# Hidden layers copied ahead of the exponential, a convolution cut in two, and finer waits, in an attention, gate and mixer kernel on one core

## The reference

```python
scores = q @ k.T / 8;  mask = scores >= the 32nd largest of its row
x = softmax(scores where mask) @ v                  # heads side by side: (4, 576, 512)

gate = sigmoid(sum over k of 5: conv_w[k] * x shifted by 4-k tokens)
x = (gate * (x @ w_val)) @ w_out

mixed = real(fft(fft(x, tokens), features));  u = x + mixed
un = (u - mean) / sqrt(var + 1e-6)
out = u + relu(un @ w_ch1) @ w_ch2                  # hidden width 2048
```

## Time and profile before

| | |
|---|---|
| median of 3 runs | 1065.74 us (1063.03 to 1066.76) |
| profiled execution, time | 1062.11 us |
| profiled execution, span | 1060.3 us |
| mean granted TensorE clock | 0.965 |
| busy TensorE matmul / weight load | 972.6 us (92%) / 830.5 us (78%) |
| busy VectorE | 832.9 us (79%) |
| busy ScalarE | 644.6 us (61%) |
| busy GpSimd | 408.1 us (38%) |

### The profile page before, as it was taken

How to read it: one execution, slowest core, us unless ns; L and a number is a source line. 1 busy time by engine, 2 the same in 40 slices (tenths; PEclk the granted TensorE clock), 3 DMA queues, 4 the chain that set the end, 5 groups by cost and what they waited for, 6 DMA issues and landing times.

```text
span 1060.3 us, 20106 instructions
## 1 busy us (share of the span) xinstructions
PE 972.6 (92%) x6784; PEld 830.5 (78%) x6784; DVE 832.9 (79%) x1809; ACT 644.6 (61%) x1421; POOL 408.1 (38%) x544
## 2 busy tenths in 40 slices
PE   4887767899999999999999999899899999999997
PEld 3565656678788898788888898688788887788896
DVE  7999999998999999989998886998998963120000
ACT  5887787766677767566677565576586761122121
POOL 2675554445433233245342323254342223443221
PEclk9987887899999999999999999999999999999999
DMA  8564656550267778401878565300677766059873
GB/s 243 176 203 158 207 170 213 191 204 23 86 244 270 279 264 284 156 4 63 289 250 264 189 221 188 128 28 23 212 260 256 255 254 213 1 187 370 282 253 128
DMA packets 84549, 203.80 MB, mean 192 GB/s; under 512 B 9056, under 2 KB 30304, under 8 KB 84448
## 3 DMA queue, kind: packets, MB, share of 16 engines
q1 hardware_dynamic: 84288, 202.22, 56.3%
q10 hardware_dynamic: 160, 0.30, 0.1%
HBM read 178.89 MB, written 23.59 MB: 191 GB/s over the span
## 4 chain that ended last, share of the span: by engine, by line
PE 71%; DVE 10%; issue 8%; ACT 7%; POOL 3%; DMA 1%; SPq 0%; ACTq 0%; DVEq 0%; POOLq 0%
PE p_m L759 18%; PE p_m L744 17%; PE p_t L597 8%; PE p_s L567 6%; PE p_t L581 5%; PE p_m L608 5%; PE p_m L638 3%; PE p_m L712 3%; DVE top L973 3%; DVE rest L984 3%; PE p_m L628 2%; ACT pT L851 2%; ACT prob L837 2%; PE p_t L601 1%; ACT s_sb L825 1%
## 5 line engine op out<-in xcount | busy, mean ns | idle before, releaser
L973 DVE MAX8 top<-rest 128x8 f32<-128x576 f32 x432 | 309.9, 745 | 0.1
L1245 POOL TENSOR_TENSOR hid_lo<-hid,hid_hi 128x256 fp32r<-128x256 f32 (+1 forms) x128 | 105.2, 822 | 307.6 <-ACT hid_hi L919 307.6
L984 DVE MATCH_REPLACE8 rest<-top,rest 128x576 f32<-128x576 f32 x288 | 213.8, 742 | 0.0
L759 PE MATMUL p_m<-w_st,hid_hi 128*128 128x512 f32 x576 | 182.4, 398 | 5.7 <-POOL hid_lo L1245 5.5
L744 PE MATMUL p_m<-un_hi,w_st 128*128 128x256 f32 (+1 forms) x1024 | 164.5, 303 | 4.7 <-ACT hid_hi L919 4.6
L825 ACT ACTIVATE s_sb<-p_s 128x576 f32<-128x576 f32 x144 | 93.1, 647 | 100.3 <-PE p_s L567 100.2
L744 PEld LDWEIGHTS p_m<-un_hi,w_st 128*128 128x128 f32 x1024 | 143.0, 188 | 12.2 <-issue 8.6
L581 PE MATMUL p_t<-id_sb,prob 128*128 128x128 f32 x720 | 108.8, 283 | 26.9 <-ACT prob L843 26.8
L597 PE MATMUL p_t<-pT,v_sb 128*64 128x128 f32 (+1 forms) x1600 | 108.6, 288 | 23.7 <-ACT pT L851 23.7
L918 ACT ACTIVATE hid<-p_m 128x256 f32<-128x256 f32 (+1 forms) x128 | 51.3, 401 | 127.0 <-PE p_m L744 124.0
L597 PEld LDWEIGHTS p_t<-pT,v_sb 128*64 128x64 f32 x1600 | 89.2, 149 | 49.3 <-ACT pT L851 29.6
(11 more groups left out here) (117 smaller groups left out, 1642.1 us busy)
## 6 DMA issues: line engine op xcount, KB each, us to landing
w_st<-w_split SPq DMA_DIRECT2D x256, 512.0 KB, 4.8
w_split<-w_st SPq DMA_DIRECT2D x32, 512.0 KB, 3.1
k_raw<-kT SPq DMA_DIRECT2D x62, 144.0 KB, 3.0
q_raw<-qT SPq DMA_DIRECT2D x60, 144.0 KB, 2.9
u<-w_ch SPq DMA_DIRECT2D x32, 256.0 KB, 3.8
v_sb<-v SPq DMA_DIRECT2D x16, 256.0 KB, 3.0
w_st<-wout_split SPq DMA_DIRECT2D x16, 256.0 KB, 4.1
out<-u SPq DMA_DIRECT2D x16, 256.0 KB, 2.4
```

Of the source, the lines that this page charges most:

```text
L759: mm = pe.matmul(mbank(j), h[i % 2][:, P * j:P * j + P], w2_st[i % NB2][:, w, :], start=f == 0 and part == 0, stop=f == FC - 1 and part == 2)
L973: found = dve.max(top[t % NK][:, 8 * n:8 * n + 8], (rest[t % 2] if n else s_sb[t % NS])[:, :])
L984: chained(dve.match_replace(rest[t % 2][:, :], top[t % NK][:, 8 * n:8 * n + 8], (rest[t % 2] if n else s_sb[t % NS])[:, :], LOWEST), t)
L1245: pool.tensor_tensor(hid_lo[i % 2][:, 0:width(b, g)], hid[:, 0:width(b, g)], hid_hi[i % 2][:, 0:width(b, g)].bitcast(F32), ALU.subtract).t ...
```

## The change

It has seven parts. (1) In slots whose first step is `ch0` n with n < 12, ScalarE does that step (the two Relu copies) ahead of `exponent`. (2) GpSimd's `deviation` of r=4 moves from step `proj` 4 to behind `hid_lo` of layer 1. (3) The convolution of c = 3 is cut into columns 0 to 383 (`FRONT`, slots 39 to 41, as soon as three fifths of `x_new` are there) and 384 to 575 (`BACK`, all five taps in slot 42). (4) `zed` 2 goes to bank 3 and waits for `gv` chunk by chunk; `sequence` g=0 takes its three operands in the order in which ScalarE copies them, each with a wait of its own. (5) `values` waits for `x_new` pair by pair. (6) Layer 1 of `ch1` goes to bank 2 in odd batches too, and `sums` of layer 0 then waits for that layer's copy before it uses bank 2. (7) `w_val` is loaded 15 slots earlier.

```diff
     if g == 0:
         return 3 if f == 1 or f >= 12 and f % 2 == 0 else 2
-    return 2 if b % 2 == 0 and f % 2 else 3
+    return 2 if (b % 2 == 0 or f == 1) and f % 2 else 3
...
+ZED_BANK = [0, 1, 3]
...
-           35: [(2, (0, 1))], 36: [(2, (2, 3))], 37: [(2, (4,))], 42: [(3, (0, 1))], 43: [(3, (2, 3, 4))]}
+WHOLE, FRONT, BACK = (0, S), (0, 3 * P), (3 * P, S)
+           39: [(3, FRONT, (0, 1))], 40: [(3, FRONT, (2, 3))], 41: [(3, FRONT, (4,))], 42: [(3, BACK, range(TAPS))]}
...
-                    if i == 2 * FC - 1:
+                    if i == FC:
                         sp.dma_start(wslot[:, :, :], w_val.rearrange("(c q) n -> q c n", q=P)).then_inc(m_wval, 16)
...
                     for k in pairs:
+                        if j == 0:
+                            pe.wait_ge(s_x, 5 * (PAIRS * b + k + 1))
...
-                        pe.wait_ge(s_x, 5 * PAIRS * (b + 1))
...
                     if m == 2:
-                        pe.wait_ge(m_gv, upto_gv(b + 1, 0))
                         for k in range(KC):
+                            pe.wait_ge(m_gv, upto_gv(b, max(2 * (k + 1), 5)))
...
-                        pe.wait_ge(m_zev, 3 * b + 3)
...
+                    for n, k in enumerate((2, 0, 1)):
+                        if g == 0:
+                            pe.wait_ge(m_zev, 3 * b + n + 1)
...
                     for j in range(len(GROUPS[b % 2][g])):
+                        if f == 0 and j == 2:
+                            pe.wait_ge(m_hev, i + 2)
...
+                    first = any(what == "ch0" and n < 12 for what, b, n in plan[s][0:1])
+                    if first:
+                        step(*plan[s][0])
                     if due(s, EXPONENT):
                         exponent(s - EXPONENT)
...
-                    for x in plan[s][0:1]:
-                        step(*x)
+                    if not first:
+                        for x in plan[s][0:1]:
+                            step(*x)
...
-                    dve.wait_ge(s_x, 5 * (p + 1))
+                    n0, n1 = part
+                    dve.wait_ge(s_x, 5 * p + (3 if part == FRONT else 5))
...
-                    elif what == "proj":
+                    elif what == "proj" and n < NR - 1:
                         deviation(b, n)
...
+                        if g == 0 and n == 1:
+                            deviation(b, NR - 1)
```

More of the change, by code:

```diff
@@ L359, in conv_due @@
         def conv_due(s):
-            return [(b, c, taps) for b in range(1, B) for c, taps in CONV_AT.get(s - NT * b, [])]
+            return [(b, *x) for b in range(1, B) for x in CONV_AT.get(s - NT * b, [])]
         def tanh_due(s):
@@ L669, in zed @@
                     if m == 2:
[L670 removed]
                         for k in range(KC):
+                            pe.wait_ge(m_gv, upto_gv(b, max(2 * (k + 1), 5)))
                             for half, c0 in enumerate((0, DM - NCOS)):
[L674 removed]
+                                mm = pe.matmul(mbank(ZED_BANK[m])[LEFT * half:LEFT * half + LEFT, 0:NCOS], gv_rows(k, 4),
                                                wfeat[:, k, c0:c0 + NCOS], start=k == 0, stop=k == KC - 1,
@@ L680, in zed @@
                         for o, (c0, c1) in enumerate(((0, NCOS), (NCOS, DM))):
-                            mm = chain(mbank(m), slice(0, P), c0, c1, [folded(k, o, m) for k in range(KC)],
+                            mm = chain(mbank(ZED_BANK[m]), slice(0, P), c0, c1, [folded(k, o, m) for k in range(KC)],
                                        [wfeat[:, k, c0:c1] for k in range(KC)])
@@ L691, in sequence @@
                     cols = slice(P * g, P * g + TCH[g])
-                    for tab, c0, c1 in ((cos_sb, 0, NCOS), (sin_sb, NCOS, DM)):
-                        mm = chain(mbank(SEQ_BANK[g]), seq_rows(b, g), c0, c1, [tab[:, k, cols] for k in range(3)],
-                                   [z[:, 0, c0:c1], z[:, 1, c0:c1], z_last[:, NCOS - (c1 - c0):NCOS]])
+                    bank = mbank(SEQ_BANK[g])[seq_rows(b, g), :]
+                    for n, k in enumerate((2, 0, 1)):
+                        if g == 0:
+                            pe.wait_ge(m_zev, 3 * b + n + 1)
+                        for tab, c0, c1 in ((cos_sb, 0, NCOS), (sin_sb, NCOS, DM)):
+                            part = z_last[:, NCOS - (c1 - c0):NCOS] if k == 2 else z[:, k, c0:c1]
+                            mm = pe.matmul(bank[:, c0:c1], tab[:, k, cols], part, start=n + c0 == 0, stop=n == 2,
+                                           skip_group_check=True)
                     mm.then_inc(m_ab, 1)
@@ L1033, in reciprocal, with conv @@
                     dve.reciprocal(rinv[:, c], rinv[:, c]).then_inc(s_rinv, 1)
-                def conv(b, c, taps):
+                def conv(b, c, part, taps):
                     p = PAIRS * b + c
-                    dve.wait_ge(s_x, 5 * (p + 1))
+                    n0, n1 = part
+                    dve.wait_ge(s_x, 5 * p + (3 if part == FRONT else 5))
                     if c == 0:
@@ L1040, in conv @@
                     for k in taps:
-                        src = x_new[p % NX][:, k:k + S]
+                        to, src = gate[:, c, n0:n1], x_new[p % NX][:, k + n0:k + n1]
                         if k == 0:
-                            dve.tensor_scalar(gate[:, c, :], src, cw_sb[:, c, 0:1], None, ALU.mult).then_inc(m_conv, 1)
+                            dve.tensor_scalar(to, src, cw_sb[:, c, 0:1], None, ALU.mult).then_inc(m_conv, 1)
                         else:
                             dve.wait_ge(m_conv, tapped[0])
-                            dve.scalar_tensor_tensor(gate[:, c, :], src, cw_sb[:, c, k:k + 1], gate[:, c, :],
-                                                     ALU.mult, ALU.add).then_inc(m_conv, 1)
+                            dve.scalar_tensor_tensor(to, src, cw_sb[:, c, k:k + 1], to, ALU.mult,
+                                                     ALU.add).then_inc(m_conv, 1)
                         tapped[0] += 1
@@ L1129, in _ @@
                         low_keys(p)
-                    for b, c, taps in conv_due(s):
-                        conv(b, c, taps)
+                    for b, c, part, taps in conv_due(s):
+                        conv(b, c, part, taps)
                     for x in plan[s][1:]:
```

12 lines of the change are left out of this document (7 added, 5 removed).

## The result

| | before | changed |
|---|---|---|
| median | 1065.19 us (1063.03 to 1066.76, 4 runs) | 1049.03 us (1045.98 to 1052.33, 4 runs) |
| ratio, 95% interval | | 0.985 (0.981 to 0.989) |
| profiled execution: time, span | 1062.11, 1060.3 us | 1052.33, 1050.6 us |
| VectorE busy | 832.9 us | 839.0 us |

The changed kernel is faster by 1.5%. Repeated with the kernel before on the same chip it gave 1048.75 us (1046.24 to 1051.45, 6 runs) against 1063.36, ratio 0.987 (0.984 to 0.989), so 14.6 to 16.2 us. The two profiled executions differ by only 9.8: the changed kernel's was the slowest of its four runs, and that of the kernel before was shorter than all four of its timed runs.

A forecast was written before the change was run, and what follows sets the result against it. VectorE and TensorE were taken to bound the kernel in turn. Terms 5.0 + 2.5 + 1.0 + 5.1 + 1.9 + 0.8 + 1.1 = 17.4, taken as 17 us, gave about 1049 us; forecast between 1045 and 1053, range 1044 to 1059.

The forecast's parts named there:

- What bounds the kernel: VectorE sets 60 to 208 us, both engines are full 268 to 422, TensorE alone counts after 886.
- Deviation, 5.0, and 1.5 of clock: TensorE's waits behind GpSimd in slots 54, 126, 89 and last batch go, 5.0 us; half clock behind slot 126, 1.5.
- Order on ScalarE, net 1.0: Hidden copies ahead of the exponential: 3.5 us gained in two-layer slots, 2.5 lost to stalls in short slots.
- Convolution, 5.1, and its 1.0 of clock: Gates of batches 1 and 2: earlier taps end ScalarE's tanh wait, saving TensorE 5.1 us, plus 1.0 of half clock.
- No stretch at half clock after 680 us: Sign expected in the changed profile: TensorE's half-clock spell behind slots 115 and 116 is gone.
- VectorE's idle time as cover: Cut's extra 0.6 us per batch is covered by VectorE's 2.5 us idle from 422 us, more in slots 111 to 113.
- Finer waits: `zed` and `sequence` start by chunk or operand: 1.9 us (bounds 0 and 3.2), about 1.3 of wait remaining in batch 1.
- The sum of the parts, given as 4.7: At 454 us, batch 1: 2.0 + 0.6 - 1.2 + 1.5 + 1.9, against 3.3 us with the last chunk still waiting.
- The rest: `values` of the last batch 0.8 us, bank 2 for `ch1` layer 1 in the last batch 1.1, earlier `w_val` nothing.
- VectorE is the bound: Rival, chance 0.13: TensorE's gains in its full stretches become waits for the top-32 search; gain about 7.6, so 1058 us.
- ScalarE did not stay blocked: Rival, chance 0.12, said ScalarE stays blocked: BACK's taps and searches keep the gate's tanh late; gain 11, so 1055 us.
- the exponential's delay did not decide: Rival, chance 0.04, said it decides: transposes stall in nearly all 24 slots; full shift costs 36 us, so 1082.

The follow-up runs named there:

- the version that leaves it out: Changed kernel with copies first only in two-hidden-layer slots, batch 1's convolution whole, bank 2 for layer 1 of `ch1` only in the last batch: 1045.59 us, ratio 0.9805.
- the kernel with the order alone: Kernel before with only ScalarE's new order, copies of the first twelve layers ahead of the exponential: 1059.80 us, ratio 0.9968.
- the two-layer order: Changed kernel with copies ahead of the exponential only in slots with two hidden layers: 1045.11 us, ratio 0.9823; on the last chip 1047.30, ratio 0.9819.
- the exponential first: Changed kernel with ScalarE's old order, exponential ahead of the hidden layer's two copies: 1050.22 us, ratio 0.988.

## Why the prediction was right, point by point

The total was right, and most of its terms were; one of the two largest, the gates, was not.

- *What bounds the kernel.* Right: every stage in which TensorE waited between slots 54 and 62, 88 and 99, 126 and 134 shrank by about its waits, and the first 208 us did not move beyond their noise. VectorE's being busy 152 of 154 us from 268 to 422 did not stop TensorE: the moved deviation alone kept all of its 2.2 us there.
- *Deviation, 5.0, and 1.5 of clock.* Measured alone 6.3 us, with the longer spell at the gate of batch 2 in its profile; its four stages sum to 7.1. Right. In slot 54, where before the sequence was deviation, then `hid_lo`, it is now the other way round: `hid_lo` of layer 0 ran at 285.57 us, that of layer 1 at 288.14, the deviation at 288.96, and no wait is left.
- *Order on ScalarE, net 1.0.* Measured 2.3 gained in batch 1 and 1.2 lost in the others, net 1.1, and 1.9 over everything from slot 42 on: right in sign and place. The agreement of the net is in part luck, since the 0.4 at the gate was not in the sum, and since the slots with one layer alone cost some 3 us and not 2.5. Slot 58's transposes wait 0.71 for the exponential, where 0.89 was worked out from the earlier trace rows:

```profile
308.33 0.19 ACT L858 ACTIVATION_READ_ACCUMULATOR prob<-prob,bias 128x1 f32 x1
...
308.57 0.77 PE L588 MATMUL p_t<-id_sb,prob 128*128 128x128 f32 x5 [0.71 <-ACT prob L858]
```

- *Convolution, 5.1, and its 1.0 of clock.* This step failed in its size. The prediction said: "ScalarE's wait goes, and with it 5.1 us of TensorE's". ScalarE's wait did shrink, and TensorE's waits at the tanh went; but the stages of the two gates (93.1 us before) shrank by 1.1 us in the execution with half-clock spells and by 4.4 in the one without, for this and the finer wait of `zed` together, where 1.9 + 4.6 = 6.5 had been worked out. Undoing the cut alone cost 0.5 us of median, which is within the noise. What the sum had too small is the wait of `zed` for VectorE's last product, once ScalarE no longer holds TensorE up: 2.57 us where 1.3 was said, and 2.36 where none was. Two terms behind that were mis-sized too. The cut costs VectorE 0.22 us a tap, not 0.12. All the convolution grew by 5.1 us (54.8 against 49.7): some 3.3 of that is the cut, worked out from the typical instructions, and the rest is taps and first products that waited longer for GpSimd. VectorE's busy time rose by 6.1 us where about 2 had been said. And the clock was counted as a gain at the gates, where the wait that remains at `zed` can bring the spell back: it did in both gates of one execution and in neither of the other. "No stretch at half clock after 680 us" therefore failed in the first.
- *VectorE's idle time as cover.* The four FRONT taps of slots 39 and 40 take 4.0 us in batch 1, more than the 2.5 that were idle. One of them alone takes 1.67, behind GpSimd. VectorE, which before stood 2.42 us waiting for TensorE's closing sums (line 1079, now 1100), comes to them 1.4 us later, counted from the start of slot 77:

```profile
424.35 1.29 DVE L1079 TENSOR_TENSOR u<-p_m,u 128x512 f32<-128x512 f32 x2 [2.42 <-PE p_m L759]
```

```profile
426.23 1.28 DVE L1100 TENSOR_TENSOR u<-p_m,u 128x512 f32<-128x512 f32 x2
```

(before and changed; slot 77 starts at 422.41 and 422.85). The last `gv` ends 30.2 us behind that start in place of 30.0: the cut did not bring it forward at all. In batch 2 it comes 1.4 us earlier, and there the cut pays.
- *Finer waits.* Right that a wait of `zed` would remain in batch 1, wrong in its size (1.3 said, 2.57 measured), and one of 2.36 in batch 2 had not been foreseen. In the last batch `zed`'s wait went (from the first matmul of `val` to that of `zed` 16.43 to 15.72 us) as said. The sum of the parts, given as 4.7, is 4.8, which changes nothing.
- *The rest.* 1.1 for the bank in the last batch: that stretch shortened by 1.6 with 0.5 of the deviation in it, right. But "in batch 1 attention stands between the two layers and nothing is gained" left out a loss: the added wait of `sums` holds TensorE 0.74 us in slot 100, since ScalarE comes to that copy only behind its attention work. 0.66 us in slots 99 to 104, shown by the version that leaves it out.
- *The rivals.* "VectorE is the bound" held, from slot 42 on, at the two gates and nowhere else. The Trainium skill (Perfetto Trace Analysis, Optimizing Scalar/DVE Operations) says that larger operations help on a saturated engine; batch 1, where VectorE was full, agrees (0.3 to 1.9 us lost by the cut), batch 2, where it had idle time ahead, gained. ScalarE did not stay blocked, and the exponential's delay did not decide: the longest new stall is 0.71 us, and the granted clock behind it stayed at 1.00.

The sum of 17 was 2 us more than the stages gave without half-clock spells (14.9) and 5 more than with them (12.1). That the median came out at 1049.0, to the microsecond as forecast, is luck: the range was right, but the medians differed by 16.2 in those runs, by 14.6 on the other chip.

## What to carry to other kernels

A wait taken from the bounding engine is worth its length only until the next producer: before counting it, ask when the last input of the next step will be ready, and which engine makes it. Putting a copy ahead of other work in a queue pays where a second consumer in the same slot waits for it and costs wherever the work behind it has less room than the shift; here doing it in 10 of 24 places gave some 3 us more than doing it in all. Price a cut instruction by a row of its own form and memory, and by the typical instruction and not the mean: mine drew a line from a form that read PSUM beside SBUF at 257 columns (0.414 us) to a mean (0.863) that taps held up by GpSimd had raised, and its fixed part came out at 0.05 where 0.22 was measured. When the mean of a group lies well above most of its members, look at what runs beside the long ones.

## What the runs showed of the hardware beyond that

Whether a wait of TensorE is followed by a spell at half clock differs between executions, and its length does not decide it. The same wait of 1.99 us in slot 54 had none behind it in the kernel before and one in the kernel with the order alone; waits of 2.57 and 2.36 us had one in one execution of the changed kernel and none in the other; 2.91 us had none in both executions of the two-layer order and one with the exponential first; and 3.62 us in slot 118 had none with all whole taps in slot 42. The spells at the gates cost 1.5 to 1.7 us when matmuls fill them, and the longer one of the kernel with the late `w_val` 3.0.

A tap of `scalar_tensor_tensor` over SBUF that nothing disturbs takes 0.82 us for 576 columns, 0.62 for 384 and 0.42 for 192. That is one line, 0.22 us and 1.04 ns a column, so every cut costs the fixed 0.22 once more. Over the 13 profiles here 115 taps took longer. Each of them met a GpSimd instruction that was still running more than 0.2 us behind the tap's start, and each ended 0.61 to 0.62 us (576 columns) or 0.41 to 0.42 us (384 columns) after that instruction's end, which is the part of the tap that grows with its columns. The tap at 415.30 above ends at 416.97, 0.42 behind GpSimd's end at 416.55. So where a tap starts against GpSimd's work decides whether it takes 0.62 or 1.67 us; this is read from the traces, and no run here was made to test it.
